# Four first-tile bias tables instead of eight, wide tables grouped in two places, and a copy of scores put between exponentials, in a fused attention and MLP kernel

## What is computed

```python
scores = matmul(q, k.T) / 8                      # 2 x 8 heads, 768 x 768
keep   = (pos_k < n_global) | (0 <= rel < n_local)    # 8 and 96 here
bias   = -slope[h] * dist                        # slope[h] = 2 ** -(h + 1)
a      = softmax(where(keep, scores + bias, -1e9))
x      = a @ v                                   # to 2 x 768 x 512
# then: x + U,V mixing over tokens, an MLP with relu (w_ch1, w_ch2), and a
# gated MLP with a 768 x 768 product over tokens (w_in, w_spatial, w_out)
```

## Time and profile before

| | |
|---|---|
| median of 3 runs | 495.94 us (495.88, 495.94, 499.2) |
| the profiled execution, its own time | 496.05 us |
| its span in the profile | 494.3 us |
| TensorE matmul busy | 488.0 us, 99% |
| VectorE, ScalarE, GpSimd busy | 312.3, 222.1, 249.6 us |
| granted TensorE clock, share of full speed | 0.999 |

### The profile page before, as it was taken

One profiled execution on the slowest core, in us unless ns is written; L12 is line 12 of the kernel. 1 busy time (PEld: TensorE's weight loads), 2 busy tenths in 40 slices (PEclk: granted clock), 3 DMA queues, 4 the chain that ended last, 5 costly groups with the idle time before them and its releaser, 6 DMA issues.

```text
span 494.3 us, 7920 instructions
## 1 busy us (share of the span) xinstructions
PE 488.0 (99%) x2786; PEld 407.4 (82%) x2786; DVE 312.3 (63%) x726; ACT 222.1 (45%) x521; POOL 249.6 (51%) x219
## 2 busy tenths in 40 slices
PE   8999999999999999999999999999999999999997
PEld 7788677887888888888888888888888888998985
DVE  5888788511279466564655656557878888878600
ACT  7988888532234633242342322415452356333121
POOL 5798566443346666855476546232885201950000
PEclk9999999999999999999999999999999999999999
DMA  8823501132222322012221020220112000001022
GB/s 240 270 88 110 191 2 44 46 113 100 67 83 105 131 85 76 16 80 86 85 87 73 13 85 2 85 64 2 64 65 112 7 0 1 1 1 47 19 91 100
DMA packets 14552, 36.27 MB, mean 73 GB/s; under 512 B 2480, under 2 KB 2480, under 8 KB 14512
## 3 DMA queue, kind: packets, MB, share of 16 engines
q1 hardware_dynamic: 12640, 32.35, 19.4%
q10 hardware_dynamic: 1872, 3.41, 1.8%
HBM read 32.61 MB, written 3.15 MB: 72 GB/s over the span
## 4 chain that ended last, share of the span: by engine, by line
PE 96%; ACT 3%; DMA 1%; issue 0%; SPq 0%; ACTq 0%
PE bank L1748 15%; PE bank L1474 13%; PE bank L1830 9%; PE bank L1680 9%; PE bank L1605 9%; PE bank L1777 9%; PE bank L1770 9%; PE bank L1848 7%; PE bank L1530 4%; PE bank L1512 4%; PE bank L1497 3%; ACT prob L1157 1%; PE bank L1544 1%; PE bank L1552 1%; DMA qk_raw<-in_qk 1%; PE bank L1577 1%
## 5 line engine op out<-in xcount | busy, mean ns | idle before, releaser
L520 POOL TENSOR_TENSOR w_slot<-stage,w_slot 128x1024 fp32r<-128x1024 f32 x30 | 73.4, 2456 | 64.8 <-ACT w_slot L1227 64.8
L918 DVE TENSOR_TENSOR uT<-bank,uT 128x512 f32<-128x512 f32 x68 | 45.8, 689 | 25.2 <-PE bank L1777 23.2
L1157 ACT ACTIVATE prob<-prob,row_min 128x256 f32<-128x256 f32 (+1 forms) x96 | 45.9, 480 | 7.5 <-DVE row_min L736 7.4
L1748 PE MATMUL bank<-u_op,s_slot 128*128 128x512 f32 x192 | 47.6, 389 | 0.0
L1680 PE MATMUL bank<-hid,w_slot 128*128 128x512 f32 x192 | 46.9, 393 | 0.0
L1605 PE MATMUL bank<-u_split,w_slot 128*128 128x512 f32 x192 | 46.5, 391 | 0.0
L1777 PE MATMUL bank<-hid,w_slot 128*128 128x512 f32 x192 | 46.1, 389 | 0.0
L1770 PE MATMUL bank<-hid,w_slot 128*128 128x512 f32 x192 | 46.1, 389 | 0.0
L956 DVE TENSOR_TENSOR part<-part,bank 128x512 f32<-128x512 f32 x40 | 27.4, 686 | 26.2 <-PE bank L1748 25.8
L1680 PEld LDWEIGHTS bank<-hid,w_slot 128*128 128x128 f32 x192 | 35.7, 188 | 8.2 <-issue 0.9
L1748 PEld LDWEIGHTS bank<-u_op,s_slot 128*128 128x128 f32 x192 | 36.0, 188 | 7.5
(11 more groups left out here) (149 smaller groups left out, 959.5 us busy)
## 6 DMA issues: line engine op xcount, KB each, us to landing
stage<-in_w_ch SPq DMA_DIRECT2D x32, 512.0 KB, 3.3
qk_raw<-in_qk SPq DMA_DIRECT2D x23, 256.0 KB, 4.5
v_all<-in_v SPq DMA_DIRECT2D x12, 256.0 KB, 4.6
out_dram<-o_stage ACTq DMA_DIRECT2D x12, 256.0 KB, 2.0
stage<-in_w_spT SPq DMA_DIRECT2D x6, 384.0 KB, 3.2
stage<-in_w_in SPq DMA_DIRECT2D x4, 512.0 KB, 4.4
stage<-in_w_out SPq DMA_DIRECT2D x2, 512.0 KB, 3.9
V_raw<-in_V SPq DMA_DIRECT2D x4, 96.0 KB, 4.4
```

Of the source, the lines that this page charges most:

```text
L520: nc.gpsimd.tensor_tensor(dst[:, LO, :], stage[n % 2][:, 0:w], dst[:, HI, :].bitcast(F32), ALU.subtract).then_inc(w_lo, 1)
L918: vec.tensor_tensor(y, y_bank(e)[:], y, ALU.add).then_inc(y_sum, 1)
L1157: last = sc.activation(prob[r][:, e, 0:w], prob[r][:, e, 0:w], ACT.Exp, bias=row_min[:, k:k + 1], scale=-1.0, accum_out=row_sum[:, q:q + 1])
L1748: last = mm(seven_bank[held][:], lhs, u_op[op][:, m, k, :], start=not more and k == 0 and p == 0, stop=k == 1 and p == 2, skip_group_check ...
```

## The change

1. **Four narrow tables.** ScalarE builds narrow tables only for heads 0, 1, 4 and 5 ahead of groups 0 and 1. The second pair of each of these groups (heads 2, 3 and 6, 7) uses the tables two heads before it. A slope two heads on is smaller by a factor of 4, so q of that pair is multiplied by 4 (`SPREAD`) when it is rounded, and the bias step divides by 4 more.
2. **Splits of tile 0 in pieces.** To scale q of one chunk alone, each instruction of 512 columns at lines 1137 and 719 becomes three: one of 256 columns (chunk c, q and k) and two of 128 (k and q of chunk c + 1). The semaphore is counted by the last of the three. On VectorE the last one is a `scalar_tensor_tensor` with the factor 4.
3. **The other four narrow tables** (heads 2, 3, 6, 7), which groups 12 and 13 need, are built one each at the end of ScalarE's steps 5, 6, 7 and 8. VectorE waits for all eight ahead of groups 12 and 13.
4. **Wide tables in two places.** Before: two tables in step -2 ahead of exps(0), two in step -1 behind exps(1), two in step 0 and two in step 1. After: four in step -2 ahead of exps(0), four in step 0 ahead of exps(2).
5. **A copy between exponentials.** ScalarE's take_probT(2) moves from the start of step 2 to step 1, between the two pairs of exps(3).

```diff
 for hq in range(2):                                  # VectorE
-    c = slice(2 * hq, 2 * hq + 2)
+    c = 2 * hq
     dve.wait_ge(qk0_hi, hq + 1)
-    vec.tensor_tensor(qk_split[:, LO, c, :, 0:P], qk_raw[0][:, c, :, :],
-                      qk_split[:, HI, c, :, 0:P].bitcast(F32), ALU.subtract).then_inc(qk0_lo, 1)
+    vec.tensor_tensor(qk_split[:, LO, c, :, 0:P], qk_raw[0][:, c, :, :],
+                      qk_split[:, HI, c, :, 0:P].bitcast(F32), ALU.subtract)
+    vec.tensor_tensor(qk_split[:, LO, c + 1, K, 0:P], qk_raw[0][:, c + 1, K, :],
+                      qk_split[:, HI, c + 1, K, 0:P].bitcast(F32), ALU.subtract)
+    vec.scalar_tensor_tensor(qk_split[:, LO, c + 1, Q, 0:P], qk_raw[0][:, c + 1, Q, :], SPREAD,
+                             qk_split[:, HI, c + 1, Q, 0:P].bitcast(F32), ALU.mult, ALU.subtract
+                             ).then_inc(qk0_lo, 1)
...
                     if g < 2:                        # VectorE, score_bias
-                        dve.wait_ge(bias0_set, heads(g, m)[1][1] + 1)
+                        dve.wait_ge(bias0_set, 2 * g + 2)
                     elif g < 4:
                         dve.wait_ge(bias_set, heads(g, m)[1][1] + 1)
+                    elif w == P:
+                        dve.wait_ge(bias0_set, H)
...
-                            bias0[:, h, :] if w == P else bias[:, h, :],
-                            -SCALE, 3.0e38, ALU.add, ALU.min, row_min[:, k:k + 1])
+                            bias0[:, h - 2 * m if g < 2 else h, :] if w == P else bias[:, h, :],
+                            -SCALE / SPREAD if g < 2 and m else -SCALE, 3.0e38, ALU.add, ALU.min, row_min[:, k:k + 1])
...
-                sc.activation(qk_split[:, HI, c, :, 0:P], qk_raw[0][:, c, :, :], ACT.Copy).then_inc(qk0_hi, 1)
+                sc.activation(qk_split[:, HI, c, :, 0:P], qk_raw[0][:, c, :, :], ACT.Copy)
+                sc.activation(qk_split[:, HI, c + 1, K, 0:P], qk_raw[0][:, c + 1, K, :], ACT.Copy)
+                sc.activation(qk_split[:, HI, c + 1, Q, 0:P], qk_raw[0][:, c + 1, Q, :], ACT.Copy, scale=SPREAD
+                              ).then_inc(qk0_hi, 1)
             act.wait_ge(dist0_set, 1)
-            for h in range(H):
+            def set_bias0(h):
                 sc.activation(bias0[:, h, :], dist0[:], ACT.Copy, scale=-(2.0 ** -(h + 1)) / SCALE
                               ).then_inc(bias0_set, 1)
+            for h in FIRST_TABLES:                   # (0, 1, 4, 5)
+                set_bias0(h)
...
                 for s in range(-2, QUADS):           # ScalarE
-                    if s >= 2:
+                    if s >= 3:
                         take_probT(s)
...
-                    if s in (-2, 0, 1):
-                        set_bias((0, None, 4, 6)[s + 2])
+                    if s in (-2, 0):
+                        set_bias(2 * s + 4)
+                        set_bias(2 * s + 6)
                     if s >= 2:
                         take_xT(s - 2, s)
-                    if 0 <= s + 2 < QUADS:
+                    if s == 1:
+                        exps(3, 0)
+                        take_probT(2)
+                        exps(3, 1)
+                    elif 0 <= s + 2 < QUADS:
                         exps(s + 2)
-                    if s == -1:
-                        set_bias(2)
+                    if s in (5, 6, 7, 8):
+                        set_bias0(FIRST_TABLES[s - 5] + 2)
```

More of the change, by code:

```diff
@@ L219, in build @@
             sem("wide_" + n) for n in ("turned", "probT", "out_ps", "o", "store", "back", "heads")]
+        SPREAD = 4.0
+        FIRST_TABLES = (0, 1, 4, 5)
         def heads(g, m):
@@ L1134, in _ @@
             for hq in range(2):
-                c = slice(2 * hq, 2 * hq + 2)
+                c = 2 * hq
                 act.wait_ge(qk_in[0][hq], 16)
-                sc.activation(qk_split[:, HI, c, :, 0:P], qk_raw[0][:, c, :, :], ACT.Copy).then_inc(qk0_hi, 1)
+                sc.activation(qk_split[:, HI, c, :, 0:P], qk_raw[0][:, c, :, :], ACT.Copy)
+                sc.activation(qk_split[:, HI, c + 1, K, 0:P], qk_raw[0][:, c + 1, K, :], ACT.Copy)
+                sc.activation(qk_split[:, HI, c + 1, Q, 0:P], qk_raw[0][:, c + 1, Q, :], ACT.Copy, scale=SPREAD
+                              ).then_inc(qk0_hi, 1)
             act.wait_ge(dist0_set, 1)
-            for h in range(H):
+            def set_bias0(h):
                 sc.activation(bias0[:, h, :], dist0[:], ACT.Copy, scale=-(2.0 ** -(h + 1)) / SCALE
                               ).then_inc(bias0_set, 1)
+            for h in FIRST_TABLES:
+                set_bias0(h)
             def set_bias(first):
```

## The result

The changed kernel takes 499.03 us (median of 22 executions, 497.97 to 499.69) against 495.94 for the kernel before (22 executions, median 495.94): ratio 1.0055, 95% interval [1.0047, 1.0064]. It is 3.1 us slower, where 0.6 us less was forecast; 499.03 lies outside the range of 494.4 to 496.3. A difference of 0.6% was, rightly, put within 1%, but its sign is the other one.

What follows compares the result with a forecast made beforehand. TensorE, with 96% of the chain, was taken as the bound, so only its start could shorten. Terms: 0.31 late, 0.54 and 0.48 gained at weigh(2), 0.09 given to the rhythm: -0.62, so 495.3 us, range 494.4 to 496.3.

Steps and rivals of the forecast that it cites:

- Splits in pieces: Tile 0 rounding and subtraction: VectorE's second half ends at 7.19 instead of 6.87; first exponential 0.17 later.
- Nothing of it counts: VectorE's later second half: TensorE's fillers end 0.2 to 0.3 later, turn(0) is wanted about 0.2 later; no cost.
- the 0.62: Net gain in us at scores(5), 19.89 instead of 20.51, and so in the whole time.
- both waits of weigh(2): TensorE's waits for VectorE's and ScalarE's copies at weigh(2) vanish: 0.54 before its start and 0.48 inside it.
- 0.31 paid for it: Delay of exps(2) and scores(4): 0.17 from VectorE's branch, 0.14 from add_eps and rounding.
- 1: ScalarE up to its copy at 18.40: all it saves counts, 1.49 earlier, 494.45 us; chance 0.08.
- 5: Later stage paced by transfers takes the gain back: nothing remains, 495.9 us; chance 0.05.
- rival 2: Ahead of the first bias step: VectorE's branch isn't tied to the rounding, 0.17 more gained, 495.15 us; chance 0.12.
- rival 3: Ahead of exps(0): VectorE's branch waits for its third piece, 0.73 late instead of 0.17, 495.9 us; chance 0.13.
- 4: Steps 5 to 8: late narrow tables delay ScalarE's copies, up to 0.20 per group, +0.18 net, 496.1 us; chance 0.07.
- The rival on the slower side: The case of late narrow tables holding up ScalarE's copies, the only one forecast slower: 496.1 us, chance 0.07.

Runs made afterwards that it cites:

- the kernel with the hold: Changed kernel, with GpSimd waiting for the end of VectorE's splits of tile 0 before its first split: 495.30 us, ratio 0.9982 to the kernel before.
- early branch, no more fillers: Changed kernel with GpSimd held until VectorE's tile 0 splits end, and VectorE's register loads and branch moved between the split halves: 495.37 us, ratio 0.9991.
- TensorE kept at work: Changed kernel with 8 more identity products on TensorE between scores(0) and scores(1), GpSimd not held: 496.82 us, ratio 1.0024 to the kernel before.
- VectorE's pieces alone: Kernel before, with VectorE's subtraction of tile 0 in three pieces and ScalarE's rounding whole: 499.92 us over five executions, ratio 1.0075.

## Why the prediction was wrong

**The step that failed** is *Splits in pieces*, for VectorE: "The second half starts at 6.34 and ends at 7.19 instead of 6.87". It starts at 6.39 and ends at 9.06. The 0.21 and 0.35 per piece were taken from rows in which VectorE reads one operand from PSUM; the splits read both from SBUF, and in the second half GpSimd is at work beside them. Alone the pieces do end at 6.95 + 0.28 = 7.23. The term missing is GpSimd's cast, subtract and cast: 9.06 - 7.23 = 1.8 us. The step asked of GpSimd only whether its tile of group 6 comes late, not what it does between 6.2 and 9, though its cast of 1.09 beside one of 0.60 was there to be seen.

The Trainium skill has this rule, and I did not weigh it. "SBUF — State Buffer", section "SBUF: two separate sides", says of VectorE and GpSimd that the port pair they share is "an **exclusive lock**, not a bandwidth split": whichever starts first has it for the whole instruction, a VectorE instruction with two SBUF inputs against a GpSimd one that reads SBUF among them. All the rows above agree: 0.42 / 0.28 / 0.28 alone, 0.78 / 1.35 / 0.69 beside GpSimd, and 0.29 for bias steps with one operand in PSUM beside the same subtract.

**"Nothing of it counts"** (the fillers) failed with it. The forecast had scores(1) follow scores(0) without a pause. With 1.76 of idle the clock went to 1.2 GHz, and that cost more (2.2 by the medians, 2.9 in the profiled executions) than the delay (1.5 and 1.2). The prediction had no term for the clock.

**What held**, as the kernel with the hold shows, forecast against measured: first bias step 7.94 / 8.00, exps(0) 8.49 / 8.55, exps(2) 13.28 / 13.35, scores(4) 16.42 / 16.49, weigh(2) in one piece 17.32 / 17.39, turn(3) 18.34 / 18.42, scores(5) 19.89 / 19.95, time 495.3 / 495.30. So the 0.62 was rightly worked out, with both waits of weigh(2) gone and 0.31 paid for it. As a difference from before it is small: of the four kernels with the change and the hold three lie at ratios of 0.9975 to 0.9982 with intervals below 1 (0.9988 or 0.9989 by the medians), the fourth (early branch, no more fillers) at 0.9991 with one that takes in 1.

**The rivals.** 1 and 5 (more, or nothing, remains): no, by the same rows. 2 and 3 (the branch): in the kernel with the hold the bias step lies 0.23 later than before, near the 0.17 forecast, where rival 2 has 0 and rival 3 has 0.73; moved ahead of the second half it lies at 7.36. In the changed kernel the queue's work (DVEq) was over at about 7.9, before the third piece began at 8.37, as this part of its chain says. So it bound nothing there, and it had not waited for that piece, as rival 3 has it:

```profile
7.00 0.32 DVEq L311
...
7.87 0.02 DVEq L740
7.89 0.48 issue
8.37 0.70 DVE qk_split L729
```

4 (late narrow tables hold the copies): the copy of step 6 in the kernel with the hold ends at 30.95 + 0.57 = 31.52, and the five periods from scores(7), at 26.87, on are 3.46 each. It did not happen. ScalarE there:

```profile
30.75 0.29 ACT L1158 ACTIVATE bias<-dist 128x128 f32<-128x128 f32 x1
30.95 0.57 ACT L1192 ACTIVATE probT<-bank 128x512 f32<-128x512 f32 x1
```

The rival on the slower side was thus the wrong mechanism. The true one, an engine beside the changed instructions, was on no list.

**What stays open.** The 22 executions of the changed kernel fall in three sets by their mean granted clock: nine at 0.995 to 0.997 (498.0 to 498.5), nine at 0.992 or 0.993 (499.2 to 499.7), and four at 1.000 (499.0 to 499.2), which are not the shortest. None of these four was profiled, and the median, 499.03, lies among them. So the 2.2 for the clock is a difference of medians of a mixed lot; the 2.90 is of one pair of traces. Some executions with a mean granted clock of 0.999 or more are also 2 to 3 us longer than others of the same kernel with the same mean (the kernel before: 498.6 to 499.4 beside 496.0; TensorE kept at work: 498.8 beside 496.7). Why stays open.

## What to carry to other kernels

Before an instruction is cut in pieces, look at what the other engines do in the same stretch. In these traces a whole VectorE instruction with both operands in SBUF kept GpSimd out until its end (a cast of 1.09 instead of 0.60), and each boundary let one GpSimd instruction in, a cast of 0.61 or a subtract of 1.32. The same operation with two lengths in one timeline (here 1.09 and 0.60) is the sign. Where the two must meet, let the engine that has time wait by a semaphore.

## What the runs showed that was not expected

- VectorE and GpSimd, both reading SBUF (VectorE with two operands), excluded each other for whole instructions: a 128 x 128 subtract took 1.35 beside a GpSimd subtract of 1.32, and 0.28 alone. One semaphore wait on GpSimd took 3.7 us off a kernel whose chain lies on TensorE for 96%.
- TensorE at full clock, idle for 0.73 and, after scores(0), for 1.76, came back at 1.2 GHz (granted 0.50) and stayed there for some 6 us. After 1.51 of idle, with VectorE's pieces alone, the clock was 0.66 from 10 to 15 us. After 0.80 it fell in one profiled execution (the early branch, 0.83 from 5 to 10 us) and the kernel with the hold, at 0.34, kept 1.00.
